# Two Fori loops of a fused attention, routing and expert kernel written out as straight code

## The chip, the core and the metric

The kernel runs on one core of one Trainium2 chip. The metric is the device time of one execution in microseconds (us). Three runs of the kernel before gave 960.48, 960.57 and 961.03 us: a median of 960.57 us.

Five engines work side by side, each through its own list of instructions: PE (matrix products; PEld is its load of weights), DVE (vector), ACT (activation), POOL (GpSimd) and SP, which only issues transfers here. They meet through semaphores: an instruction adds to one, and another waits until it has reached a value.

## The reference, cut to what matters

```python
# 1: linear attention with decay; r, k, v: (4, 8, 768, 48)
for t in range(S):
    cur = einsum('bhd,bhe->bhde', u * kt, vt)
    y[:, :, t] = einsum('bhd,bhde->bhe', rt, state + cur)
    state = w * state + einsum('bhd,bhe->bhde', kt, vt)
x = y.transpose(0, 2, 1, 3).reshape(3072, 384)

# 2: each token goes to one of 8 experts, best logit first, 384 tokens per expert
logits = x @ w_gate
for idx in argsort(-logits.flatten()):
    tok, e = idx // E, idx % E
    if assigned[tok] >= 0 or counts[e] >= cap: continue
    assigned[tok] = e; counts[e] += 1
for e in range(8):
    out[mask_e] = relu(x[mask_e] @ w1[e]) @ w2[e]      # w1: 384x1024, w2: 1024x384

# 3: a bilinear layer; w_a, w_b: 384x1536, w_out: 1536x384
return ((out @ w_a) * (out @ w_b)) @ w_out
```

## The kernel before, in words

**Attention.** The tokens are cut into 24 tiles of 128 (4 batches of 6). SP loads r, k and v of a tile three tiles ahead, and between them pieces of the third layer's weights (`raw`). Per tile PE makes scores (L981), turns the next tile (L957) and the last result (L965), makes the state's update (L991), the product with the scores (L999), the gate's logits (L971) and the product with the state (L1005). DVE scales and masks, POOL makes `ktok`, `ruk`, `sfade` and `dv` and, with ACT, splits the `raw` weights into an upper and a lower part (`w_all`). All four call the helper `all_tiles` (L300), which puts tile 0 ahead, tiles 1 to 18 in a loop of three passes of six, and tiles 19 to 23 behind it. SP does not use it: its list is written out.

**Routing.** The search for the first expert's tokens (24 products of L1026 and one of L1032, six times, with DVE between them) stands behind the attention, outside any loop. That for expert i+1 is spread between the products of expert i (`routing` on PE; `route_keys` and what follows on DVE, L636 to L766).

**Experts.** One call of `expert(i, ...)` takes one expert through its two layers and the bilinear layer. PE: L1069 (first layer, later the products with w_a and w_b), L1112 (second layer), L1143 (last product). Each result leaves in two parts: ACT writes the upper (`upper_hidden` L909, L922, L925), DVE the lower (`lower_hidden` L780, L807, L810). Meanwhile POOL gathers the next expert's weights by row number (`rows_i`, L681; L461, L465) into `wst` and takes off the upper part (L478); ACT makes the upper part of the first six pieces (L904), between its other work, in order.

**What the loops contain.** PE and DVE run experts 0 to 5 in one loop body and write out experts 6 and 7. ACT and POOL run seven passes in the loop and write out the last. In a loop body the pass number is a register, so a wait that grows from pass to pass is met by computing the value first (`REGISTER_ALU`, or `ISA` where the value is moved) and waiting for the register. The order of the work on each engine is that of the code; no scheduler moves it.

Of the kernel before, what the change touches and what calls it, by code (L numbers as in the profile page):

```python
# [16 lines left out]
def attention_moe_bilinear(nc, r, k, v, w, u, w_gate, w1, w2, w_a, w_b, w_out, out, x_rows):  # L17
    B, H, S, DH = r.shape
    D, E = w_gate.shape
# [32 lines left out]
    with ctx:  # L52
# [250 lines left out]
        def all_tiles(engine, tile):  # L303


            tile(0, 0, False)
            with engine.Fori(0, B - 1) as b:
                for j in range(1, TPB + 1):
                    tile(b, j, True)
            for j in range(1, TPB):  # L310
                tile(B - 1, j, False)
# [52 lines left out]
        def _(pool):  # L364
# [46 lines left out]
            def tile(b, j, in_loop):  # L411
# [20 lines left out]
                if in_loop and j >= 2:  # L432
                    for c, count, piece, cols in raw_pieces(j - 1):
# [7 lines left out]
                                   ALU.mult).then_inc(dv_ready, 1)  # L441

            all_tiles(pool, tile)


# [34 lines left out]
            def prepare(m, first):  # L480


                pool.wait_ge(rows_ready, m + 1)
                for k in range(CHUNKS + 2):
                    if k < CHUNKS:
                        gather_weights(m, k)
                    if k >= 2 and not (first and k - 2 in BY_DVE):
                        split_weights(m, k - 2, first)
                    if k == (TOKENS_AT_0 if first else TOKENS_AT):
                        pool.wait_ge(ids_ready, m + 1)  # L490
                        pool.wait_ge(xg_turned, 1 + m * DC)
                        pool.sem_inc(pool_go, 1)
                        for t in range(CT):
                            pool.indirect_dma_start(xg[:, t, :], None, x_rows,
                                                    bass.IndirectOffsetOnAxis(ap=ids_next[:, t:t + 1], axis=0)
                                                    ).then_inc(xg_landed[t], 16)

            def store(i):
                pool.wait_ge(now_ready, i + 1)
                for t in range(CT):  # L500
                    pool.wait_ge(os_ready, 1 + i * CT + (t + 1))
                    pool.sem_inc(pool_go, 1)
                    pool.indirect_dma_start(out, bass.IndirectOffsetOnAxis(ap=ids_now[:, t:t + 1], axis=0),  # L503
                                            os_[:, t, :], None).then_inc(o_stored, 16)
                pool.wait_ge(o_stored, i * (16 * CT) + 16 * CT)
                pool.sem_inc(o_flushed, 1)

            prepare(0, True)
            with pool.Fori(0, E - 1) as i:
                prepare(i + 1, False)  # L510
                store(i)
            store(E - 1)
# [2 lines left out]
        def _(dve):  # L515
# [53 lines left out]
            def tile(b, j, in_loop):  # L569
# [25 lines left out]
                if j >= 1:  # L595
# [3 lines left out]
                                  ALU.add).then_inc(x_ready, 1)  # L599

            all_tiles(dve, tile)


# [173 lines left out]
            def lower_hidden(i, f):  # L777

                dve.wait_ge(hs_hi, i * FC + (f + 1))
                dve.scalar_tensor_tensor(hs2[:, f % 2, 1, :], ring[f % 2][:, 0:CAP], 0.0,  # L780
                                         hs2[:, f % 2, 0, :].bitcast(F32), ALU.max, ALU.subtract
                                         ).then_inc(hs_lo, 1)
# [69 lines left out]
                dve.tensor_tensor(lo, src, hi.bitcast(F32), ALU.subtract).then_inc(w_split, 1)  # L852
            assert made[0] == CHAIN
            lower_hidden(0, 0)
            with dve.Fori(0, E - 2) as i:
                expert(i, True, True)
            expert(E - 2, True, False)
            expert(E - 1, False, False)
# [2 lines left out]
        def _(act):  # L861
# [8 lines left out]
            def tile(b, j, in_loop):  # L870
# [7 lines left out]
                if in_loop:  # L878
                    for c, count, piece, cols in raw_pieces(j):
# [5 lines left out]
                               ).then_inc(lg_ready, 1)  # L885

            all_tiles(act, tile)


# [16 lines left out]
            def upper_hidden(i, f):  # L906

                act.wait_ge(h_done, i * FC + (f + 1))
                act.activation(hs2[:, f % 2, 0, :], ring[f % 2][:, 0:CAP], ACT.Relu).then_inc(hs_hi, 1)  # L909

            def expert(i, more):
                for f in range(1, FC):
                    upper_hidden(i, f)
                for c in range(DC):
                    act.wait_ge(yt_done, i * DC + (c + 1))
                    act.activation(act2[:, 0, c, :], acc[c][:, 0:CAP], ACT.Copy).then_inc(yt_hi, 1)
                act.wait_ge(raw_lo, RAW_PIECES)
                for c in range(FFC):
                    act.wait_ge(a_part, i * FFC + (c + 1))

                    act.wait_ge(gs_lo, 1 + i * FFC + max(c - 1, 0))
                    act.activation(ga[:, c % 2, :], ring[2 * (c % 2)][:, 0:CAP], ACT.Copy).then_inc(as_ready, 1)  # L922

                    act.wait_ge(g_ready, i * FFC + (c + 1))
                    act.activation(gs2[:, c % 2, 0, :], ga[:, c % 2, :], ACT.Copy).then_inc(gs_hi, 1)  # L925
                    if more and c >= ACT_FROM:
                        for k in range(2 * (c - ACT_FROM), 2 * (c - ACT_FROM) + 2):
                            if k in BY_ACT:
                                upper_weights(i + 1, k)
                if more:  # L930
                    upper_tokens(i + 1)
                    upper_hidden(i + 1, 0)
                act.wait_ge(o_flushed, 1 + i)
                for t in range(CT):
                    act.wait_ge(o_done, i * CT + (t + 1))
                    act.activation(os_[:, t, :], acc[t][:, 0:D], ACT.Copy).then_inc(os_ready, 1)  # L936
# [5 lines left out]
                    act.wait_ge(raw_lo, RAW_PIECES)  # L942
                upper_weights(0, k)
            upper_hidden(0, 0)
            with act.Fori(0, E - 1) as i:
                expert(i, True)
            expert(E - 1, False)

# [1 line left out]
        def _(pe):  # L950
# [135 lines left out]
            def first_up(i):  # L1086

                for c in range(DC):
                    pe.wait_ge(w_split, 1 + i * CHUNKS + (c + 1) * (F // WIDE))
                    pe.wait_ge(xgt_lo, 1 + i * DC + (c + 1))  # L1090
                    for a, b in ((0, 0), (0, 1), (1, 0)):
                        last = pe.matmul(ring[0][:, 0:CAP], w1_2[:, a, c, 0:P], act2[:, b, c, :],  # L1092
                                         start=(c == 0 and (a, b) == (0, 0)),
                                         stop=(c == DC - 1 and (a, b) == (1, 0)))
                last.then_inc(h_done, 1)
# [87 lines left out]
                route_numbers(0, part)  # L1183
            turn_tokens(0)
            first_up(0)
            with pe.Fori(0, E - 2) as i:
                expert(i, True, True)
            expert(E - 2, True, False)
            expert(E - 1, False, False)
# [30 lines left out]
```

## Time and profile before

| | |
|---|---|
| median of 3 runs | 960.57 us |
| the profiled execution | 960.47 us, of which 958.7 us is the span from first to last instruction |
| PE busy | 900.8 us (94%) |
| DVE, POOL, ACT busy | 509.3, 470.3 and 218.8 us |
| chain that ended last | PE 92%, DVE 3%, POOL 2%, DMA 1%, issue 1% |
| mean granted TensorE clock | 0.967 |

Busy shares and the chain are means over stages: attention fills the first 180 us, the first routing goes on until about 231 us, and the experts take the rest.

### The profile page before, as it was taken

The page shows a single profiled execution, that of the slowest core. Times are in us where ns is not written, and L with a number is a line of the kernel's source. Part 1 is how long each engine was busy: PE and PEld are TensorE (multiplying, and loading weights), DVE is VectorE, ACT ScalarE, POOL GpSimd, SP SyncE. Part 2 cuts the span into 40 slices and gives each one's busy share as a digit, 9 for nine tenths or more (in the row PEclk, how much of TensorE's full clock was granted, in tenths as well). Part 3 has the DMA queues.
Part 4 walks back from the last instruction along what each step waited for, and adds up shares of the span by engine and source line. Part 5 has one row for each costly group of instructions (what it writes and reads, how often), then busy time and mean ns, then how long its engine had stood idle before and what let it go on. Part 6 is the DMA issues. An engine that isn't in the chain of part 4 may idle for free.

```text
span 958.7 us, 17931 instructions
## 1 busy us (share of the span) xinstructions
PE 900.8 (94%) x6581; PEld 864.6 (90%) x6581; DVE 509.3 (53%) x1238; ACT 218.8 (23%) x454; POOL 470.3 (49%) x491
## 2 busy tenths in 40 slices
PE   5999999625999999999999999999999999999995
PEld 5999999614999999999999999999999999999995
DVE  6777677576555456465636563656455532432221
ACT  0212120002113211322222223223312232222221
POOL 5988897216406731771178037604750673277001
PEclk9999999756999999999999999999999999999998
DMA  5785754003002200220121012101210121122000
GB/s 104 210 220 115 194 124 105 26 22 111 25 2 75 75 33 33 66 57 25 33 82 52 13 44 79 57 0 55 77 49 0 66 77 38 34 83 66 1 1 25
DMA packets 92782, 61.19 MB, mean 64 GB/s; under 512 B 78800, under 2 KB 83536, under 8 KB 92752
## 3 DMA queue, kind: packets, MB, share of 16 engines
q0 software_dynamic: 11008, 34.61, 11.8%
q1 hardware_dynamic: 77872, 21.45, 9.8%
q10 hardware_dynamic: 3872, 4.72, 1.4%
q8 instruction: 20, 0.33, 0.1%
q14 instruction: 10, 0.08, 0.0%
HBM read 51.33 MB, written 9.44 MB: 63 GB/s over the span
## 4 chain that ended last, share of the span: by engine, by line
PE 92%; DVE 3%; POOL 2%; issue 1%; DMA 1%; ACT 0%; SPq 0%; POOLq 0%; DVEq 0%; ACTq 0%
PE bank L1069 39%; PE bank L1143 16%; PE bank L1112 11%; PE bank L981 4%; PE bank L999 4%; PE bank L1026 3%; PE bank L957 2%; PE bank L1005 2%; PE bank L1125 2%; PE bank L991 2%; PE bank L1092 2%; PE bank L971 2%; PE bank L1129 1%; PE bank L965 1%; PE bank L1060 1%
## 5 line engine op out<-in xcount | busy, mean ns | idle before, releaser
L1069 PE MATMUL bank<-act,w_all 128*128 128x384 f32 x1584 | 298.4, 338 | 0.0
L1069 PEld LDWEIGHTS bank<-act,w_all 128*128 128x128 f32 x1584 | 274.4, 188 | 1.1
L461 POOL DMA_INDIRECT wst<-in_moe_w,rows_i x48 | 52.2, 1087 | 274.7 <-DVE rows_i L681 217.3
L1143 PE MATMUL bank<-w_all,gs 128*128 128x384 f32 x864 | 168.2, 338 | 0.3 <-DVE gs L810 0.3
L478 POOL TENSOR_TENSOR w<-wst,w 128x384 fp32r<-128x384 f32 (+1 forms) x106 | 131.0, 1236 | 43.6 <-ACT w L904 37.9
L1143 PEld LDWEIGHTS bank<-w_all,gs 128*128 128x128 f32 x864 | 149.6, 188 | 2.1 <-DVE gs L810 1.6
L807 DVE TENSOR_TENSOR ga<-ga,bank 128x384 f32<-128x384 f32 x96 | 53.1, 554 | 140.5 <-PE bank L1069 90.0
L1112 PE MATMUL bank<-hs,w 128*128 128x384 f32 x576 | 111.4, 339 | 0.6 <-DVE hs L780 0.6
L1112 PEld LDWEIGHTS bank<-hs,w 128*128 128x128 f32 x576 | 99.9, 188 | 1.4 <-issue 0.9
L1069 PE MATMUL bank<-act,w 128*128 128x384 f32 x504 | 99.0, 339 | 0.0
L465 POOL DMA_INDIRECT wst<-in_moe_w,rows_i x64 | 64.1, 1002 | 50.4 <-POOL w L478 35.8
L1069 PEld LDWEIGHTS bank<-act,w 128*128 128x128 f32 x504 | 87.8, 188 | 0.9
L925 ACT ACTIVATE gs<-ga 128x384 fp32r<-128x384 f32 x96 | 50.5, 526 | 157.3 <-DVE ga L807 157.3
L780 DVE SCALAR_TENSOR_TENSOR hs<-bank,hs 128x384 fp32r<-128x384 f32 x64 | 35.6, 557 | 92.6 <-ACT hs L909 89.0
L810 DVE TENSOR_TENSOR gs<-ga,gs 128x384 fp32r<-128x384 f32 x96 | 53.8, 560 | 56.8 <-ACT gs L925 56.8
L922 ACT ACTIVATE ga<-bank 128x384 f32<-128x384 f32 x96 | 46.7, 486 | 134.8 <-PE bank L1069 101.7
L909 ACT ACTIVATE hs<-bank 128x384 fp32r<-128x384 f32 x64 | 31.5, 492 | 170.9 <-PE bank L1069 153.5
L503 POOL DMA_INDIRECT out<-os_,ids_now x24 | 24.0, 1002 | 69.2 <-ACT os_ L936 63.2
L904 ACT ACTIVATE w<-wst 128x512 fp32r<-128x512 f32 (+1 forms) x50 | 30.4, 621 | 92.4 <-DMA wst<-in_moe_w,rows_i 92.2
L1026 PEld LDWEIGHTS bank<-mask_mem,want 128*8 128x8 bf16 x1008 | 28.9, 85 | 24.1 <-DVE mask_mem L630 15.3
L981 PE MATMUL bank<-rs,ks 128*128 128x128 f32 x384 | 49.0, 282 | 0.0
L1026 PE MATMUL bank<-mask_mem,want 128*8 128x41 bf16 x1008 | 35.4, 184 | 13.1 <-DVE mask_mem L630 13.1
(165 smaller groups left out, 1141.5 us busy)
## 6 DMA issues: line engine op xcount, KB each, us to landing
rt<-in_r SPq DMA_DIRECT2D x24, 192.0 KB, 3.0
kt<-in_k SPq DMA_DIRECT2D x24, 192.0 KB, 4.0
vt<-in_v SPq DMA_DIRECT2D x24, 192.0 KB, 4.1
x_rows<-xs ACTq DMA_DIRECT2D x24, 192.0 KB, 3.4
raw<-in_moe_w_a SPq DMA_DIRECT2D x3, 768.0 KB, 6.2
raw<-in_moe_w_b SPq DMA_DIRECT2D x3, 768.0 KB, 6.5
raw<-in_moe_w_out SPq DMA_DIRECT2D x3, 768.0 KB, 7.7
wst<-in_moe_w,rows_i POOLq DMA_INDIRECT x112
```

The lines of the kernel that those rows point to most:

```text
L461: pool.indirect_dma_start(wst[:, k % STAGES, :], None, w1_rows, bass.IndirectOffsetOnAxis(ap=rows_i[:, k:k + 1], axis=0)).then_inc(wst_lan ...
L465: pool.indirect_dma_start(wst[:, k % STAGES, 0:D], None, w2_rows, bass.IndirectOffsetOnAxis(ap=rows_i[:, k:k + 1], axis=0)).then_inc(wst_l ...
L478: pool.tensor_tensor(lo, src, hi.bitcast(F32), ALU.subtract).then_inc(w_split, 1)
L807: dve.tensor_tensor(ga[:, c % 2, :], ga[:, c % 2, :], ring[2 * (c % 2) + 1][:, 0:CAP], ALU.mult).then_inc(g_ready, 1)
L810: dve.tensor_tensor(gs2[:, c % 2, 1, :], ga[:, c % 2, :], gs2[:, c % 2, 0, :].bitcast(F32), ALU.subtract).then_inc(gs_lo, 1)
L922: act.activation(ga[:, c % 2, :], ring[2 * (c % 2)][:, 0:CAP], ACT.Copy).then_inc(as_ready, 1)
L925: act.activation(gs2[:, c % 2, 0, :], ga[:, c % 2, :], ACT.Copy).then_inc(gs_hi, 1)
L981: last = pe.matmul(pA[g][:, a, :], ks[:, a, g, :], rs[:, two, a, :], start=True, stop=True)
L1026: last = pe.matmul(pCnt, want[:, j, :], mask[:, j, :], start=(j == 0), stop=(j == NT - 1))
L1069: last = pe.matmul(dst, wt(a), mv(b), start=(n == 0 and (a, b) == (0, 0)), stop=(n == len(pairs) - 1 and (a, b) == (1, 0)))
L1112: last = pe.matmul(acc[c][:, 0:CAP], w2_2[:, a, f, c * P:c * P + P], hs2[:, f % 2, b, :], start=(f == 0 and (a, b) == (0, 0)), stop=(f == ...
L1143: last = pe.matmul(acc[t][:, 0:D], gs2[:, c % 2, a, t * P:t * P + P], wo2[:, b, c, :], start=(c == 0 and (a, b) == (0, 0)), stop=(c == FFC ...
```

## The change

The four uses of `Fori` become Python's `for`, so that the bodies are laid out once per pass and every number in them is a constant.

```diff
 def all_tiles(engine, tile):
             tile(0, 0, False)
-            with engine.Fori(0, B - 1) as b:
+            for b in range(B - 1):
                 for j in range(1, TPB + 1):
                     tile(b, j, True)
             for j in range(1, TPB):
@@ pool
-            with pool.Fori(0, E - 1) as i:
+            for i in range(E - 1):
                 prepare(i + 1, False)
                 store(i)
@@ dve
-            with dve.Fori(0, E - 2) as i:
+            for i in range(E - 2):
                 expert(i, True, True)
@@ act
-            with act.Fori(0, E - 1) as i:
+            for i in range(E - 1):
                 expert(i, True)
@@ pe
-            with pe.Fori(0, E - 2) as i:
+            for i in range(E - 2):
                 expert(i, True, True)
```

In the built programs PE has 2423 instructions before and 6162 now (a matrix product counted once), DVE 677 and 1421, POOL 310 and 764, ACT 259 and 617, SP 125 in both.

The first place is PE at the end of the attention loop's body, tile 6 on to tile 7. Before:

```order
L989 REGISTER_ALU
L991 MATMUL bank<-vt,ktok 128x96 [waits ktok_ready]
L991 MATMUL bank<-vt,ktok 128x96 x3
L996 REGISTER_ALU
L999 MATMUL bank<-vt,am 128x48 [waits x_ready,am_ready]
L999 MATMUL bank<-vt,am 128x48 x7
L971 MATMUL bank<-gate_w,xt 128x8 [waits xt_ready]
L971 MATMUL bank<-gate_w,xt 128x8 x2
L307 REGISTER_ALU
L307 COMPARE_AND_BRANCH
```

Now, at the same place:

```order
L991 MATMUL bank<-vt,ktok 128x96 [waits ktok_ready]
L991 MATMUL bank<-vt,ktok 128x96 x3
L999 MATMUL bank<-vt,am 128x48 [waits x_ready,am_ready]
L999 MATMUL bank<-vt,am 128x48 x7
L971 MATMUL bank<-gate_w,xt 128x8 [waits xt_ready]
L971 MATMUL bank<-gate_w,xt 128x8 x2
L981 MATMUL bank<-rs,ks 128x128 [waits am_ready,scaled]
```

The register work and the branch are gone, and the next tile's scores (L981) follow at once. The matrix products and their order are the same.

The second place is DVE at the start of an expert: `route_keys` (L639 to L651) for the next expert, then the lower part of the hidden values (L780). Before:

```order
L639 TENSOR_TENSOR lm<-logit,lid 128x192
L622 ISA
L640 TENSOR_REDUCE key<-lm 128x24 [waits dve_step]
L622 REGISTER_ALU
L643 TENSOR_SCALAR code<-key 128x24 [waits dve_step]
L644 TENSOR_TENSOR lm<-lm,key 128x192
L622 REGISTER_ALU
L645 TENSOR_TENSOR code<-code,key 128x24 [waits dve_step]
L646 TENSOR_TENSOR want<-lm,is_open 128x192
```

Now, at the same place:

```order
L639 TENSOR_TENSOR lm<-logit,lid 128x192
L640 TENSOR_REDUCE key<-lm 128x24 [waits dve_step]
L643 TENSOR_SCALAR code<-key 128x24 [waits dve_step]
L644 TENSOR_TENSOR lm<-lm,key 128x192
L645 TENSOR_TENSOR code<-code,key 128x24 [waits dve_step]
L646 TENSOR_TENSOR want<-lm,is_open 128x192
```

Nothing has changed places; the same operations wait for the same semaphores, without register work between them.

## Rows read from the trace of the kernel before

**Rows 1.** The page's chain that ended last, share of the span by engine.

```profile
PE 92%; DVE 3%; POOL 2%; issue 1%; DMA 1%; ACT 0%; SPq 0%; POOLq 0%; DVEq 0%; ACTq 0%
```

**Rows 2.** Waits of PE from 239 us on, summed over the rest.

```profile
PE bank L1112 <- DVE hs L780: 0.6, 1, 0.6
PE bank L1143 <- DVE gs L810: 0.3, 1, 0.3
```

**Rows 3.** Windows of one expert's length: length, busy time per engine, PEclk, DMA share, GB/s.

```profile
258.83:350.20 91.37, 91.37 (x656) 86.71 (x655) 50.86 (x132) 23.21 (x48) 42.82 (x42) 1.00 0.16 48
350.20:441.59 91.39, 91.39 (x656) 86.71 (x655) 50.85 (x132) 23.21 (x48) 42.82 (x42) 1.00 0.16 47
441.59:533.15 91.56, 91.56 (x656) 86.73 (x655) 50.02 (x132) 23.21 (x48) 42.51 (x42) 1.00 0.16 47
804.15:887.83 83.68, 83.68 (x504) 82.58 (x504) 30.31 (x71) 23.23 (x47) 41.56 (x42) 1.00 0.17 53
```

**Rows 4.** DMA queues of the whole run: packets, MB, share of 16 engines.

```profile
q8 instruction: 20, 0.33, 0.1%
q14 instruction: 10, 0.08, 0.0%
```

**Rows 5.** DMA queues, window 258.83 to 350.20.

```profile
q8 instruction: 4, 0.07, 0.3%
```

**Rows 6.** DMA queues, window 350.20 to 716.27; no other queue is listed.

```profile
q0 software_dynamic: 5504, 17.31, 15.5%
```

**Rows 7.** DMA queues, window 20 to 62 in the attention.

```profile
q1 hardware_dynamic: 19440, 7.47, 69.1%
q8 instruction: 3, 0.05, 0.5%
```

**Rows 8.** Timeline: start, length, engine, line, operation, [idle before]. Short routing products, in the loop and written out.

```profile
289.49 0.10 PEld L1042 LDWEIGHTS bank<-tot,before 128*128 128x128 bf16 x1 [0.16 <-issue]
332.50 0.65 PEld L1026 LDWEIGHTS bank<-mask_mem,want 128*8 128x8 bf16 x24 [0.25 <-issue]
830.51 0.10 PEld L1042 LDWEIGHTS bank<-tot,before 128*128 128x128 bf16 x1 [0.16 <-issue]
```

**Rows 9.** Timeline of the attention: starts of tiles 7, 8, 13 and 14.

```profile
61.02 2.03 PE L981 MATMUL bank<-rs,ks 128*128 128x128 f32 x16
68.31 1.98 PE L981 MATMUL bank<-rs,ks 128*128 128x128 f32 x16
102.62 2.03 PE L981 MATMUL bank<-rs,ks 128*128 128x128 f32 x16
104.96 0.42 PEld L957 LDWEIGHTS bank<-ident,rt 128*128 128x128 f32 x4 [0.51 <-DMA vt<-in_v]
110.44 1.75 PE L981 MATMUL bank<-rs,ks 128*128 128x128 f32 x14
```

**Rows 10.** Timeline of expert 0: DVE's `route_keys` beside POOL's split, and PE behind them.

```profile
236.26 0.70 DVE L645 TENSOR_TENSOR code<-code,key 128x24 int32<-128x24 int32 x1
237.00 1.11 POOL L478 TENSOR_TENSOR w<-wst,w 128x384 fp32r<-128x384 f32 x1
237.26 0.88 DVE L647 TENSOR_SCALAR code<-code 128x24 int32<-128x24 int32 x1
239.34 1.53 PEld L1112 LDWEIGHTS bank<-hs,w 128*128 128x128 f32 x9 [0.87 <-issue]
```

**Rows 11.** The same DVE operation in the first routing, where POOL is idle.

```profile
185.79 0.18 DVE L645 TENSOR_TENSOR code<-code,key 128x24 int32<-128x24 int32 x1
```

**Rows 12.** Timeline of expert 2: a gather that lands, ACT, then DVE and PE behind it.

```profile
491.00 0.63 ACT L904 ACTIVATE w<-wst 128x512 fp32r<-128x512 f32 x1 [3.25 <-DMA wst<-in_moe_w,rows_i]
493.80 1.52 PEld L1143 LDWEIGHTS bank<-w_all,gs 128*128 128x128 f32 x9 [0.26 <-DVE gs L810]
```

**Rows 13.** Window just before the clock's rise; columns as in rows 3.

```profile
232.00:234.00 2.00, 2.00 (x8) 2.00 (x7) 1.17 (x3) 0.53 (x2) 0.94 (x1) 0.50 0.05 18
```

**Rows 14.** A piece of the chain at the low clock: start, length, engine, line, count.

```profile
230.76 3.23 PE bank L1092 x9
```

## The prediction

> **What bounds the kernel now.** I read the chain that ended last first: 92% of the span is PE [rows 1]. The second view is the list of PE's waits. After 239 us the whole expert stage holds two waits, 0.6 and 0.3 us [rows 2]. So a change that only makes sequencers lighter can win no more than the few places where PE is late, plus the time in which PE is busy by the record but paced by its own instruction stream. The third view looks for the latter: windows of one expert's length. In each window of the loop PE is busy for its whole length, 91.37, 91.39 and 91.56 us, and in the written-out expert 6 for 83.68 us of 83.68 [rows 3]. Last I read the DMA queues, for the instruction packets, because more code is the one thing that the change adds.
>
> **The change part by part.**
>
> *Branches.* Of PE's branches that are taken back, two go in the attention (after tiles 6 and 12) and five in the expert loop. What they cost now is read off passes that contain one. The windows of rows 3 each hold one back edge of PE (near 326, 417 and 508 us), and PE is idle in none of them. Tile 7, the first after a back edge, starts at 61.02 and the next at 68.31, 7.29 us apart with no idle time put down to PE [rows 9]. Value 0. Bound: what rows 2 and 9 leave, under 0.1 us each.
>
> The trace shows instruction packets only where code is met for the first time: the window 258.83 to 350.20 has 4 packets on q8 [rows 5], and the next four passes list no instruction queue at all [rows 6]. The Trainium skill (Runtime: NRT & Kernel Launch, Instruction fetch mechanics) says that a taken branch whose target lies outside the fetched window stalls until its page is brought in, and counts this as a reason to unroll. By that rule the loop should have a packet and a stall in each pass; the trace doesn't agree, since the passes are repeated without any packet. What it would give if it did hold is the first rival.
>
> *Register work and waits on registers.* On PE it stands ahead of the short routing products. Those are preceded by a pause of 0.25 us of the weight load for L1026, in the loop [rows 8]. Is it the register? L1042 is the control, since it is in the loop at 289.49 and written out at 830.51: the pause is 0.16 us in both [rows 8]. I take 0 for the register, and give the pause to the change from long to short products. The 0.09 us between 0.25 and 0.16 has no control, as L1026 and L1032 exist written out only in the first routing, where they wait for DVE. Bounds: 0 to -0.09 us x 12 x 6 experts = -6.5 us; 0 is the nearer, because the control shows none.
>
> On DVE the register work stands between the steps of `route_keys`. In expert 0 this is where PE is late: L780 waits behind them, and PE's weight load for L1112 has stood idle for 0.87 us [rows 10]. But what stretches the steps there is not registers: L645 took 0.70 us and L647 0.88 beside POOL's split at 237.00 [rows 10], and L645 takes 0.18 us where POOL is idle [rows 11]. Written-out code keeps POOL's split at the same place. Value 0; bounds 0 and -0.9, the whole wait. On ACT and POOL register work hides under PE, which is what they wait for.
>
> *The two places where PE waits for something else.* (a) Tile 13 takes 110.44 - 102.62 = 7.82 us where tile 7 took 7.29: 0.5 us is lost to the late landing of a `vt` load, with `raw` loads queued before it [rows 9]. That load is issued when tile 11's `dv` is done, behind POOL's and ACT's splits of `raw`, which lose a register step each. I let them come some tenths earlier and the 0.5 us go: -0.5. Bounds -0.5 and, if an instruction packet now stands in front of the load, +1.1 (the price of a packet is worked out below). (b) From expert 2 on a pass is 91.56 and not 91.38: in it PE waits 0.26 us for DVE's `gs`, which waits for ACT, which stood in its queue behind a weight piece whose gather landed at about 491.0 [rows 12, 3]. Some 0.18 us in each of four passes, 0.7 in all. The start of the gathers depends on DVE's chain, which gets slightly shorter. I take a third of it, -0.2; bounds -0.7 and 0.
>
> *More code to fetch.* PE has 2423 instructions in the program before and 6162 after. Its queue should be q8, with 20 packets [rows 4]; by the ratio some 51 of 16 KB after, and q14 some 22 in place of 10. That is 31 x 16 KB + 12 x 8 KB = 0.6 MB beside 61 MB: as bandwidth nothing. As a stall: in the window 258.83 to 350.20 the body is met for the first time, with 4 packets on q8, and PE loses 0.02 us less than in the pass without packets; expert 6, also new code, has PE busy without a gap; and tiles 1 to 6 run at full pace with 3 packets on q8 while the loads keep the DMA engines at 69.1% [rows 3, 5, 7]. So fetching ahead covers it. As contention: 4 packets take 0.3% of 16 engines in 91.37 us, 4.4 us, so 1.1 us each [rows 5]. A gather that meets one on its DMA engine lands up to that much later, and the one of rows 12 has no slack left. ACT stands idle 3.25 us for it [rows 12]; 4 packets in 91 us fall into such a stretch in about one pass of seven, and by half of their length on average: 5 passes x 1/7 x 0.55 = +0.4. Not each shares the gather's engine, so I take +0.3.
>
> *Sum:* branches 0, registers 0, tile 13 -0.5, gathers -0.2, packets +0.3 = -0.4 us. The profiled execution took 960.47 us (span 958.7, some 1.8 around it, which doesn't change); the sum gives **960.1 us**. The median of the runs shown is 960.57, 0.1 above that execution, within their spread.
>
> **The rivals.**
>
> *Branches are dear after all.* Two back edges in the attention and five in the expert loop, each with one packet of 1.1 us to wait for: -7.7, 952.8 us. For it: nothing in the rows; PE is idle at none of the seven. 2%.
>
> *Waits on registers pace PE.* The 0.09 us of the short products goes, -6.5, and with it 953.6 us. For it: the pause is longer just at the products that exist only in the loop. Against it: L1042 in the loop. 5%.
>
> *Packets delay the gathers.* Place: ACT's L904, which waits for the gather and holds `ga` and `gs` behind it, in passes 1 to 5, which have no packets now [rows 6, 12]. Price: 1.1 us per pass if the packet of each pass always stands before that gather, 5 x 1.1 = 5.5, less the 0.7 gained elsewhere: 965.3 us. The passes are equally long, but a packet comes every 250 or so instructions and a pass isn't a whole number of them, so the place shifts; it decides from three meetings in five, 3 x 1.1 - 0.7 = +2.6. Against it: expert 0 met four packets at no cost, and expert 6 is level too. 8%.
>
> *The change doesn't do what it says:* if it left waits on registers, the time would be that of before; it would not be told from my forecast.
>
> **How the numbers follow.** My forecast has 83%, the rivals 2, 5 and 8, and 2 are left for what I don't see. 0.2%, or 1.9 us, is about what a measurement of this kernel can tell from no change; that is 958.6 to 962.5. Within the forecast the terms' bounds are -0.5 to +1.1 for tile 13, -0.9 to 0 for expert 0, -0.7 to 0 for the gathers. To these comes PE's clock: the granted clock was 0.50 until about 234 us, and nine products took 3.23 us there [rows 13, 14], while nine take 9 x 83.68 / 504 = 1.5 us at the full level [rows 3]; if it rises one such group sooner or later, the time moves by 1.7 either way. Together these make 958.4 to 961.9, the range, outside which the rivals lie. Faster by over 0.2%: 0.02 + 0.05 + 0.03 from the forecast's lower end = 0.10. Slower: 0.08. Within: 0.82.
>
> **What would show it.** Right: 50 or so packets on q8; passes of 91.3 to 91.6 us with PE busy throughout; the pause before L1042 0.16 and before L1026 still 0.25 us; tile 13 near 7.3. Wrong: a pause of 0.16 before L1026 (the second rival); PE waits for DVE's `gs` of 1 us in several passes (the third); PE idle where a packet lands.

## The result, and the profile after

The changed kernel is slower, by little: 962.56 us median against 960.48 for the kernel before on the same chip (15 runs each), ratio 1.0023 with a 95% interval of 1.0015 to 1.0031, which is 1.4 to 3.0 us. I had forecast 960.1. The profiled execution took 962.83 us against 960.47, so it shows 2.36 us to explain.

I read the same views in the same order. First the queues of the whole run and the chain that ended last, from the page:

```profile
q8 instruction: 52, 0.85, 0.4%
q14 instruction: 23, 0.19, 0.1%
...
PE 88%; DVE 4%; POOL 2%; issue 2%; DMA 2%; ACT 1%; POOLq 0%; DVEq 0%; ACTq 0%
```

The packets came as worked out (52 and 23 for the forecast 51 and 22; before 20 and 10 [rows 4]). The chain has left PE for 4% more of the span than before [rows 1]. Where it did so, the windows of one expert's length tell. Each begins at the same place of a pass, some 22.5 us behind an expert's first L1112, and is named after the expert in which it begins; columns as in rows 3:

```profile
258.67:350.24 91.57, 91.57 (x655) 86.74 (x655) 50.21 (x132) 23.20 (x48) 42.82 (x42) 1.00 0.17 48
350.24:441.83 91.59, 91.56 (x655) 86.71 (x655) 50.84 (x132) 23.20 (x48) 42.74 (x42) 1.00 0.16 48
...
716.35:806.09 89.74, 88.11 (x580) 84.86 (x581) 40.54 (x103) 23.11 (x47) 42.01 (x42) 1.00 0.16 49
806.09:890.25 84.16, 83.68 (x505) 82.54 (x504) 30.62 (x71) 23.21 (x47) 42.17 (x42) 1.00 0.18 52
```

The same window of expert 5 before, for the third of these (for the fourth it is in rows 3, 83.68):

```profile
716.27:804.15 87.88, 87.88 (x581) 84.88 (x581) 39.49 (x103) 23.12 (x47) 41.78 (x42) 1.00 0.16 49
```

Expert 5 starts 0.08 us later than before (716.35 against 716.27) and ends 1.94 later. Expert 6 adds 0.48. So hardly anything is spread over the loop: one pass is 1.86 us longer, with PE idle in it for 1.63, and the next is 0.48 longer. The list of PE's waits for 239 to 961 us names what it waited for:

```profile
PE bank L1143 <- DVE gs L810: 1.7, 3, 0.9
PE bank L1092 <- DVE act L774: 0.7, 1, 0.7
```

Before, the first of these was 0.3 us and the second wasn't there; the 0.6 us of L1112 in rows 2 is gone now. The next rows are the timeline of expert 5 after the change, from the gather of ACT's sixth and last piece of weights to the product that is late (start, length, engine, line, operation, idle before and what ended it):

```profile
761.59 1.74 POOL L461 DMA_INDIRECT wst<-in_moe_w,rows_i  x1 [0.81 <-POOL w L478]
...
766.73 0.63 ACT L904 ACTIVATE w<-wst 128x512 fp32r<-128x512 f32 x1 [4.21 <-DMA wst<-in_moe_w,rows_i]
767.27 0.47 ACT L922 ACTIVATE ga<-bank 128x384 f32<-128x384 f32 x1
767.77 0.56 DVE L807 TENSOR_TENSOR ga<-ga,bank 128x384 f32<-128x384 f32 x1 [3.10 <-ACT ga L922]
...
768.91 0.56 DVE L810 TENSOR_TENSOR gs<-ga,gs 128x384 fp32r<-128x384 f32 x1 [0.59 <-ACT gs L925]
...
769.52 1.52 PEld L1143 LDWEIGHTS bank<-w_all,gs 128*128 128x128 f32 x9 [1.24 <-DVE gs L810]
```

The same ACT instruction before, on ACT's timeline:

```profile
765.61 0.63 ACT L904 ACTIVATE w<-wst 128x512 fp32r<-128x512 f32 x1 [3.18 <-DMA wst<-in_moe_w,rows_i]
```

The gather was issued at 761.59, and at 761.52 before. ACT began 5.14 us behind it (766.73), before 4.09, so the piece is 1.05 us late; `ga`, `gs` and PE stand behind it. In that stretch the DMA view of the changed kernel has an instruction packet of PE's queue. The first row is of the window 761.0 to 767.2, the second of 763.5 to 764.0, which has nothing else in it:

```profile
q8 instruction: 1, 0.02, 1.2%
```

```profile
q8 instruction: 1, 0.02, 15.1%
```

15.1% of 16 engines for 0.5 us is 1.2 us of one engine. By the single packets of the trace it starts at 763.92, 0.15 us ahead of the gather's first data; these took 2.18 us from first to last, where the other six passes of this kernel took 1.2 to 1.65.

The second loss follows at the end of the same pass. First the changed kernel, then the one before:

```profile
780.39 1.01 POOL L478 TENSOR_TENSOR w<-wst,w 128x384 fp32r<-128x384 f32 x1
780.41 1.40 DVE L810 TENSOR_TENSOR gs<-ga,gs 128x384 fp32r<-128x384 f32 x1 [0.59 <-ACT gs L925]
...
782.40 1.53 PEld L1092 LDWEIGHTS bank<-act,w 128*128 128x128 f32 x9 [1.00 <-POOL w L478]
```

```profile
779.33 0.56 DVE L810 TENSOR_TENSOR gs<-ga,gs 128x384 fp32r<-128x384 f32 x1 [0.59 <-ACT gs L925]
779.42 0.82 POOL L476 CAST w<-wst 128x384 fp32r<-128x384 f32 x1
...
780.32 1.01 POOL L478 TENSOR_TENSOR w<-wst,w 128x384 fp32r<-128x384 f32 x1
780.47 1.52 PEld L1092 LDWEIGHTS bank<-act,w 128*128 128x128 f32 x9 [0.16 <-issue]
```

PE, ACT and DVE come 1 us late to the end of the pass, POOL doesn't. Its subtraction now starts 0.02 us ahead of DVE's instead of 0.99 behind it, and DVE's takes 1.40 us in place of 0.56. PE's weight load stands for 1.00 us in place of 0.16. With the piece's 1.05 that is 1.05 + 0.84 = 1.89, the pass's 1.86. The wait list gives the same by the matmuls, 0.9 and 0.7 us, the window's 1.63 of idle PE.

### The profile page after: what moved, and what is told of

It reads as the page before. It is cut to its first block, busy times and chain, and to the rows that moved or that the text cites. A ratio compares the mean times of both kernels' runs of the same rounds, so it can differ in the third digit from the quotient of the medians.

```text
span 961.1 us, 16277 instructions
## 1 busy us (share of the span) xinstructions
PE 902.4 (94%) x6581; PEld 866.0 (90%) x6581; DVE 512.0 (53%) x1238; ACT 218.8 (23%) x454; POOL 471.8 (49%) x491
## 4 chain that ended last, share of the span: by engine, by line
PE 88%; DVE 4%; POOL 2%; issue 2%; DMA 2%; ACT 1%; POOLq 0%; DVEq 0%; ACTq 0%
PE bank L1069 36%; PE bank L1143 14%; PE bank L1112 11%; PE bank L981 5%; PE bank L999 4%; PE bank L1026 3%; PE bank L957 2%; PE bank L1005 2%; PE bank L1125 2%; PE bank L991 2%; PE bank L971 2%; PE bank L1092 2%; POOL w L478 1%; DMA wst<-in_moe_w,rows_i 1%; PE bank L1129 1%
## 5 line engine op out<-in xcount | busy, mean ns | idle before, releaser
L1069 PE MATMUL bank<-act,w_all 128*128 128x384 f32 x1584 | 298.5, 339 | 0.0
L1069 PEld LDWEIGHTS bank<-act,w_all 128*128 128x128 f32 x1584 | 274.4, 188 | 1.2
L1143 PE MATMUL bank<-w_all,gs 128*128 128x384 f32 x864 | 168.2, 338 | 1.7 <-DVE gs L810 1.7
L1143 PEld LDWEIGHTS bank<-w_all,gs 128*128 128x128 f32 x864 | 149.7, 188 | 3.9 <-DVE gs L810 3.8
L1112 PE MATMUL bank<-hs,w 128*128 128x384 f32 x576 | 111.3, 339 | 0.0
L1112 PEld LDWEIGHTS bank<-hs,w 128*128 128x128 f32 x576 | 100.0, 188 | 0.6
L1069 PE MATMUL bank<-act,w 128*128 128x384 f32 x504 | 99.9, 342 | 0.0
L1069 PEld LDWEIGHTS bank<-act,w 128*128 128x128 f32 x504 | 88.7, 190 | 0.9
L810 DVE TENSOR_TENSOR gs<-ga,gs 128x384 fp32r<-128x384 f32 x96 | 55.4, 577 | 56.8 <-ACT gs L925 56.8
L780 DVE SCALAR_TENSOR_TENSOR hs<-bank,hs 128x384 fp32r<-128x384 f32 x64 | 35.6, 557 | 91.8 <-ACT hs L909 91.3
L1026 PEld LDWEIGHTS bank<-mask_mem,want 128*8 128x8 bf16 x1008 | 28.9, 85 | 24.1 <-DVE mask_mem L630 16.0
L981 PE MATMUL bank<-rs,ks 128*128 128x128 f32 x384 | 49.3, 284 | 0.0
L1026 PE MATMUL bank<-mask_mem,want 128*8 128x41 bf16 x1008 | 35.4, 184 | 13.1 <-DVE mask_mem L630 13.1
```

Source lines behind the costliest of these rows:

```text
L810: dve.tensor_tensor(gs2[:, c % 2, 1, :], ga[:, c % 2, :], gs2[:, c % 2, 0, :].bitcast(F32), ALU.subtract).then_inc(gs_lo, 1)
L981: last = pe.matmul(pA[g][:, a, :], ks[:, a, g, :], rs[:, two, a, :], start=True, stop=True)
L1026: last = pe.matmul(pCnt, want[:, j, :], mask[:, j, :], start=(j == 0), stop=(j == NT - 1))
L1069: last = pe.matmul(dst, wt(a), mv(b), start=(n == 0 and (a, b) == (0, 0)), stop=(n == len(pairs) - 1 and (a, b) == (1, 0)))
L1112: last = pe.matmul(acc[c][:, 0:CAP], w2_2[:, a, f, c * P:c * P + P], hs2[:, f % 2, b, :], start=(f == 0 and (a, b) == (0, 0)), stop=(f == ...
L1143: last = pe.matmul(acc[t][:, 0:D], gs2[:, c % 2, a, t * P:t * P + P], wo2[:, b, c, :], start=(c == 0 and (a, b) == (0, 0)), stop=(c == FFC ...
```

## The experiments

Theory A: the loss is one PE packet in front of that gather, in one pass, and the collision at the pass's end behind it. Rival B: the written-out code itself slows an engine. Lines in kernels with an edit can be up to three off: L1142 and L1145 are L1143, L1091 and L1094 are L1092, L1068 is L1069, L813 is L810. A ratio compares with the kernel before on the same chip, whose median was 960.16 us for the first four experiments, 959.26 for the next four and 959.97 for the last four; none of the differences is over 0.3% but that of the kernel with 480 waits, so read the intervals.

**PE's expert loop back to a loop, all else written out.**

```
-            for i in range(E - 2):
+            with pe.Fori(0, E - 2) as i:
                 expert(i, True, True)
```

> The changed kernel, with PE's expert loop alone put back as a loop; DVE, ACT, POOL and the attention stay written out. Theory A (PE's instruction packets delay a weight gather that ACT, DVE and PE then wait for): hardly any q8 packets in the passes of the search experts, no wait of PE for gs over 0.35 us there, ratio to before 1.000 (960.5 us). Theory B (the written-out DVE, ACT and POOL code shifts the gathers or their users so that PE waits): the loss stays, ratio 1.002 (962.5 us). Theory C (spread of the gathers alone, no packets in it): also unchanged from the written-out kernel, 1.002.

Measured: 960.14 against 960.16 us, ratio 0.9997 (0.9987 to 1.0007). Its page and its expert 5:

```profile
q8 instruction: 26, 0.43, 0.2%
...
715.15:803.19 88.04, 88.04 (x580) 84.87 (x581) 39.66 (x103) 23.14 (x47) 41.60 (x42) 1.00 0.17 49
```

With the 26 packets gone the long pass is gone, PE busy for all of it. The loops of ACT, DVE and POOL and the whole attention stay written out and cost nothing.

**PE's expert loop alone written out.**

```
-            with pe.Fori(0, E - 2) as i:
+            for i in range(E - 2):
                 expert(i, True, True)
```

> The kernel before, with PE's expert loop alone written out; all other loops stay. Theory A: some 47 packets on q8, PE late at L1143 by about 1 us in one or two passes, ratio 1.001 to 1.002 (961.5 to 962.5 us). Theory B: as before, 1.000 (960.5 us).

Measured: 962.61 us, ratio 1.0015 (1.0006 to 1.0025). Waits of PE's weight load between 625 and 890 us:

```profile
PEld bank L1143 <- DVE gs L810: 2.1, 2, 1.0
PEld bank L1092 <- POOL w L478: 2.0, 2, 1.0
```

PE's code alone is enough. Here experts 5 and 6 are both hit (89.51 and 85.21 us): packets start 0.42 us ahead of the gather's data in the one and 0.01 behind its start in the other.

**The attention alone written out.**

```
-            with engine.Fori(0, B - 1) as b:
+            for b in range(B - 1):
```

> The kernel before, with the attention loop alone written out on all four engines; the expert loops stay. Theories A and B both put the loss into the experts: ratio 0.999 to 1.000 (960.0 to 960.5 us), tile 13 shorter by 0.3 us, no pause at other tiles. A rival D puts it into the attention (packets beside the loads, a later rise of the clock): 1.001 to 1.002.

Measured: 960.43 us, ratio 1.0004 (0.9994 to 1.0013): nothing. Its expert 6 took 84.33 us, 0.65 more than before, without an instruction packet within 6 us of that gather. In the waits of PE's weight load between 625 and 890 us the first row is what stands at this pass's end:

```profile
PEld bank L1092 <- POOL w L478: 1.0, 1, 1.0
PEld bank L1143 <- DVE gs L810: 0.7, 2, 0.4
```

DVE's subtraction took 1.36 us there, behind POOL's. So the collision of POOL and DVE at the end of a pass also comes without a packet.

**All written out, and ACT's sixth piece later.** If theory A holds, the cure is slack and not fewer packets. The piece is split after product group 8 in place of 7.

```
-                    if more and c >= ACT_FROM:
-                        for k in range(2 * (c - ACT_FROM), 2 * (c - ACT_FROM) + 2):
-                            if k in BY_ACT:
-                                upper_weights(i + 1, k)
+                    if more:
+                        for k in {5: (0, 1), 6: (2, 3), 7: (4,), 8: (5,)}.get(c, ()):
+                            upper_weights(i + 1, k)
```

> The changed kernel, but ACT makes the upper part of weight piece 5 one product later (after the upper parts of product 8 instead of those of product 7), so that a late gather of it holds nothing back. Theory A: q8 still has 52 packets, PE's waits for gs at L1143 vanish (0.3 us in most passes, 1 us in one), ratio 0.999 to 1.000 (959.5 to 960.5 us). Theory D (loss elsewhere than at this gather): 1.0015 to 1.002 (962 to 962.5 us). A knock-on on POOL (piece 5 is split 3 us later) would show as a wait of PE at L1092 for POOL or DVE, up to 1 us per pass: 1.005.

Measured: 958.35 us, ratio 0.9978 (0.9969 to 0.9987). Expert 5, and ACT in it, `ga` and then the sixth piece:

```profile
714.25:801.95 87.70, 87.70 (x581) 84.90 (x581) 39.35 (x103) 23.14 (x47) 41.83 (x42) 1.00 0.16 50
```

```profile
760.29 0.47 ACT L922 ACTIVATE ga<-bank 128x384 f32<-128x384 f32 x1
...
764.77 0.63 ACT L904 ACTIVATE w<-wst 128x512 fp32r<-128x512 f32 x1 [1.25 <-DMA wst<-in_moe_w,rows_i]
```

The packet still comes, 0.36 us after the gather's first data, and the data take 2.41 us, the longest of all these kernels. But that `ga` is 4.48 us ahead of the piece and PE loses nothing: same 52 packets, same meeting, no loss. By the ratio it is 2.1 us faster than the kernel before, more than theory A explains (below).

**The changed kernel again.**

> The changed kernel itself once more, as the neighbour of the next three on one chip. Theory A (a PE instruction packet in front of the gather of weight piece 5): ratio 1.002 again, and the pass with the packet 47 to 49 us after its start (expert 5) 1 to 2 us longer than the others. Theory C (gathers spread on their own): 1.002 too, but the long pass is another one.

Measured: 961.08 against 959.26 us, ratio 1.0018 (1.0009 to 1.0027). Expert 5 is the long one again:

```profile
715.92:805.33 89.41, 88.12 (x581) 84.86 (x581) 40.39 (x103) 23.16 (x47) 41.68 (x42) 1.00 0.16 49
```

Its packet starts 0.20 us ahead of the gather's data, in the first run 0.15. Two profiled executions of one program thus met in the same place, 0.05 us apart. Expert 6 took 83.43 us this time, in the first profile 84.16. The executions without a profile can't tell: the changed kernel's first fifteen spread from 960.09 to 963.69 us, the kernel before's from 958.84 to 961.23, so it isn't excluded that some of them escape the meeting.

**The code moved by idle instructions.** 240 waits on PE that are already fulfilled, before the first tile, and 240 before the first tokens; then another kernel with 56, only before the tokens.

```
+            for _ in range(240):
+                pe.wait_ge(s_cpool, CP_CAUSAL)
             turn_tokens(0)
```

> The changed kernel with 240 more PE instructions that do nothing (waits already met) where PE is idle: half before the attention, half while PE waits for the first tokens. A packet brings 256 instructions, so all packets come later by 16 instructions, some 1.4 us against the work: the one of expert 5 at 48.8 us in place of 47.4, behind the gather's last data, and none of experts 1 to 5 lies at 46.4 to 48.6. Theory A: no wait of 1 us for gs in experts 1 to 5, ratio 1.000 to 1.001 (960.3 to 961.3 us). Theories B and C: as the changed kernel, 1.002 or more (the extra instructions can only add).

> The changed kernel with 28 more PE instructions that do nothing, while PE waits for the first tokens. All packets of the experts come some 2 us earlier against the work: that of expert 4 moves from 49.7 to 47.7 us after its start, into the gather of piece 5, that of expert 5 to 45.4, before it. Theory A: the long pass is expert 4 and no longer 5, ratio 1.001 to 1.003. Theories B and C: expert 5 stays the long one (B), or no rule (C).

Measured: 976.52 us, ratio 1.0178 (1.0165 to 1.0192), with 480; 961.67 us, ratio 1.0022 (1.0012 to 1.0033), with 56. Of the first kernel two of PE's waits before 300 us, and its expert 5; of the second, experts 5 and 6:

```profile
PE bank L957 <- issue: 17.5, 1, 17.5
PE bank L1062 <- issue: 13.3, 1, 13.3
```

```profile
732.66:820.38 87.72, 87.72 (x580) 84.89 (x581) 39.43 (x103) 23.16 (x47) 41.87 (x42) 1.00 0.16 50
```

```profile
715.12:804.23 89.11, 88.11 (x580) 84.86 (x581) 40.43 (x103) 23.15 (x47) 41.41 (x42) 1.00 0.16 50
804.23:889.38 85.15, 83.82 (x504) 82.54 (x504) 31.19 (x71) 23.25 (x47) 41.89 (x42) 1.00 0.17 52
```

The expectations count instructions (240 and 28) where the kernels got twice as many waits (480 and 56); whether two such waits make one instruction isn't shown, the first kernel has one packet more on q8 (53). I missed the total of the first, and the ratio of the second fell into what I expected, but not its long passes. The first wait was 6.6 us and the second 5.9 in the changed kernel; the idle instructions themselves cost that kernel its 17 us, so its ratio says nothing. From the window of expert 0 to the end of that of expert 6, though, it took 628.43 us, the changed kernel 631.58 and the one before 629.00: no pass is hit; the packets come 1.21 us (expert 5) and 0.77 us (expert 6) behind the gather's first data. With 56 the packet of expert 5 moved by only 0.4 us, to 0.58 ahead, so expert 5 stayed long, and the next one moved into expert 6's gather (0.43 ahead). The place decides, then; how far a given number of instructions moves it I could not forecast.

The meetings of all these kernels beside each other, from the single packets of the trace. "Packet" is its start from the gather's first data, "data" the time from first to last, "PE idle" the time without a matrix product in the 50 us from the pass's first gather on:

```
kernel, expert                    packet   data   PE idle
changed, 5                        -0.15    2.18   1.63
changed, 6                        +1.65    1.65   0.48
changed again, 5                  -0.20    2.01   1.29
changed again, 6                  +1.07    1.19   0.00
PE alone written out, 5           -0.42    2.03   1.38
PE alone written out, 6           +0.01    2.06   1.41
56 waits more, 5                  -0.58    1.78   1.00
56 waits more, 6                  -0.43    2.01   1.33
480 waits more, 5                 +1.21    1.25   0.00
480 waits more, 6                 +0.77    1.12   0.00
changed, 4                        +2.24    1.26   0.00
PE in a loop, 5                   none     1.36   0.00
late piece, 5                     +0.36    2.41   0.00
late piece, 6                     +1.45    1.45   0.00
late piece again, 5               +0.06    2.11   0.00
late piece, PE alone out, 5       +0.14    2.20   0.00
late piece, PE alone out, 6       -0.46    2.10   0.00
```

A packet that starts between 0.6 us ahead of the first data and 0.4 behind goes with data times of 1.8 to 2.4 us, ten times out of ten. In all other passes of all 14 traces they are 1.1 to 1.65, mostly under 1.4, and passes without any packet near reach 1.6 too. In nine of the ten meetings, and in no other pass, three or four of the gather's 80 packets stand by themselves, over 0.25 us behind the others. That fits one of the 16 DMA engines being held by the instruction packet; the trace doesn't name a packet's engine, so this last step is inferred. With the piece late, PE doesn't notice: four hits, no idle time.

**Before, with the late piece alone.** Is the gain of the best version that of the late piece?

> The kernel before, loops and all, with ACT's piece 5 one product later, as in e4. Theory A: the small waits for gs (0.2 to 0.3 us in most passes) go: ratio 0.998 to 0.999 (958.4 to 959.5 us), and the two kernels with the later piece are equal within 0.1%, so that with slack at this gather written-out code costs nothing. If written-out code had a cost or a gain of its own, the two would differ by it: Theory E (constants win 1 us that the packets hid): 0.999 to 1.000 here, over 0.1% above e4.

Measured: 959.91 us, ratio 1.0007 (0.9998 to 1.0016). No gain, and my expectation failed. Its five passes from the window of expert 0 on took 91.5 to 91.6 us where the written-out kernel's took 91.3 (one 91.37). Locating the 0.3 us took the timeline at the end of a pass, here of expert 3:

```profile
595.11 0.51 POOL L476 CAST w<-wst 128x384 fp32r<-128x384 f32 x1
595.23 0.81 DVE L810 TENSOR_TENSOR gs<-ga,gs 128x384 fp32r<-128x384 f32 x1 [0.59 <-ACT gs L925]
...
595.97 1.47 DVE L774 TENSOR_TENSOR act<-bank,act 128x384 fp32r<-128x384 f32 x3
596.62 1.54 PEld L1091 LDWEIGHTS bank<-act,w 128*128 128x128 f32 x9 [0.41 <-issue]
```

POOL's copy starts 0.12 us ahead of DVE's subtraction, which then takes 0.81 us in place of 0.56, and PE waits 0.41 in place of 0.16. It is so at all seven ends of passes, with 0.77 to 0.91 us for the subtraction. In the written-out kernel with the late piece the copy comes 0.1 us behind it at six of seven, and the subtraction takes 0.56. It is the collision of expert 5 above on a smaller scale, and the trace gives its rule: in all 21 places of the 14 traces where POOL's copy or subtraction was running when this subtraction started, and ran on for more than 0.2 us, DVE ended 0.41 to 0.43 us after POOL did (here POOL at 595.62, DVE at 596.04; in expert 5 above POOL at 781.40, DVE at 781.81). DVE doesn't share, it waits for the end of POOL's operation. Two theories remained for the 0.3 us: this order (O), or the back edges (L). Four kernels on one chip tell them apart.

**The same, with the order forced.**

```
                 pool.sem_inc(pool_go, 1)
+                if k == 7 and not first:
+                    pool.wait_ge(gs_lo, 1 + m * FFC)
+                    pool.sem_inc(pool_go, 1)
                 src, hi, lo = parts_of(k)
```

> The looped kernel with ScalarE's late sixth piece, and one wait more: GpSimd begins its copy of the eighth piece of weights (CAST, L476) only when VectorE has ended its last subtraction of the pass (L810). In the run without this wait the copy came 0.1 us ahead of that subtraction at every end of a pass, the subtraction took 0.77 to 0.91 us in place of 0.56, the gap before TensorE's first L1091 of the pass was 0.55 to 0.70 in place of 0.35, and passes took 91.57 to 91.59. Theory O (the order of these two at the pass's end makes the 0.3 us per pass, not the loops' back edges): passes of 91.3, gap 0.35, ratio 0.998 against before. Rival L (the loops' own branches and register operations make it): passes stay 91.55 to 91.6 although the gap goes to 0.35 or not, ratio 1.000 to 1.001.

Measured: 958.47 against 959.97 us, ratio 0.9983 (0.9975 to 0.9992). A pass of the loop, and its end:

```profile
441.18:532.49 91.31, 91.31 (x655) 86.77 (x655) 51.77 (x132) 23.20 (x48) 43.08 (x42) 1.00 0.15 47
```

```profile
595.35 0.56 DVE L813 TENSOR_TENSOR gs<-ga,gs 128x384 fp32r<-128x384 f32 x1 [0.59 <-ACT gs L928]
...
596.08 0.51 POOL L479 CAST w<-wst 128x384 fp32r<-128x384 f32 x1 [0.61 <-DVE gs L813]
...
596.50 1.53 PEld L1094 LDWEIGHTS bank<-act,w 128*128 128x128 f32 x9 [0.16 <-issue]
```

All passes of the loop are 91.29 to 91.31 us, with all loops in place. Theory O holds: on top of the late piece, one wait on POOL is worth 0.3 us a pass, and back edges nothing. The wait without the late piece was not run.

**Late piece, with PE's loop alone written out; late piece, with PE's loop alone kept; the best version again.**

> The looped kernel with ScalarE's late sixth piece and TensorE's expert loop alone written out (q8 near 46 packets). If the 0.3 us per pass of the kernel with everything written out is TensorE's own back edge: passes of 91.3, ratio 0.998. If it is the order of GpSimd's copy and VectorE's subtraction at the end of a pass: whichever order this version falls into decides, 91.3 with VectorE first, 91.55 to 91.6 with GpSimd first. In both theories no pass of 89 us for the expert after the last search, since the late piece is hidden.

> Everything written out and the sixth piece late, but TensorE's expert loop a loop again (q8 near 26 packets). If TensorE's back edge costs the 0.3 us per pass: passes of 91.57, ratio 1.000. If the loops of the other engines did: passes of 91.3, ratio 0.998. If it is the order of copy and subtraction: the passes with VectorE first 91.3, the others 91.55 to 91.6, with either ratio.

> The same kernel as the one with everything written out and the late sixth piece, again, on this chip: ratio 0.998 (0.997 to 0.999) against before, VectorE first at every end of a pass, passes of 91.3, q8 52 packets. If it was chance or the chip, 0.999 to 1.001 and passes of 91.55 to 91.6.

Measured: 958.18 us, ratio 0.9982 (0.9973 to 0.9991); 958.40 us, 0.9981 (0.9973 to 0.9990); 958.70 us, 0.9984 (0.9976 to 0.9993). A pass of the kernel with PE's loop written out, then of the one that keeps it:

```profile
440.55:531.85 91.30, 91.30 (x656) 86.75 (x655) 50.75 (x132) 23.23 (x48) 42.74 (x42) 1.00 0.16 48
```

```profile
439.45:530.75 91.30, 91.30 (x655) 86.76 (x655) 51.77 (x132) 23.20 (x48) 42.74 (x42) 1.00 0.16 48
```

So with slack for the sixth piece and the good order, it is the same whether PE's loop is written out or not, and whether the others' are. In all three DVE is first at every end. At one end (411 us of the kernel with PE's loop) the subtraction took 0.73 us all the same, and the pass, from L1091 to L1091, 91.48. So the order of the starts isn't all of it, but the subtraction's length and the pass's go together here too. Why the loop kernel with the late piece fell into the other order, and these three did not, is open; each was profiled once, the best version twice.

## Why the prediction was wrong

*Branches and registers, 0.* Right. The pause before L1026 is 0.25 us in the changed kernel too, and before L1042 0.16:

```profile
277.09 0.65 PEld L1026 LDWEIGHTS bank<-mask_mem,want 128*8 128x8 bf16 x24 [0.25 <-issue]
...
289.32 0.10 PEld L1042 LDWEIGHTS bank<-tot,before 128*128 128x128 bf16 x1 [0.16 <-issue]
```

Both rivals that rested on sequencers fall, and the loop with forced order shows it from the other side: 91.3 us a pass with the back edge. (Their times were not counted from one base: 952.8 and 965.3 start from the 960.5 of the kernel before, 953.6 from the forecast.)

The Trainium skill's rule that a taken branch beyond the fetched window stalls (Runtime: NRT & Kernel Launch, Instruction fetch mechanics) is not seen at PE's back edge: with it and without it a pass takes 91.30 us, by the windows of the kernels with the late piece. But the prediction drew too much from it. The same section of the Trainium skill gives PE's instruction memory room for 2048 instructions, in blocks of 256, beside the window of two pages. A pass of PE is about five such blocks, by the 26 packets that five passes more bring, so by the size of the memory the body fits and no packet is due in a repeated pass. The trace agrees with that size, and not with a window of two pages.

*Tile 13, -0.5.* Half of it: the wait for `vt` is 0.21 us in place of 0.51, and the tile takes 7.53 in place of 7.82. Nothing of it is left at the routing: tile 13 itself starts 0.68 us later than before (103.30 and 102.62), since tile 0 took 7.6 us in place of 6.7, and near 200 us the two kernels are within 0.02 us of each other.

```profile
105.35 0.42 PEld L957 LDWEIGHTS bank<-ident,rt 128*128 128x128 f32 x4 [0.21 <-DMA vt<-in_v]
```

*Expert 0 and the clock.* The wait of 0.87 us [rows 10] is gone, yet expert 0's window starts only 0.16 us earlier (258.67 and 258.83). The two go together. The granted clock rose later. The first pair of rows is of the kernel before, the second of the changed one, each a window and then the first layer's products (L1069) that the rise falls into:

```profile
234.00:235.50 1.50, 1.50 (x9) 1.50 (x9) 0.93 (x3) 0.49 (x1) 0.99 (x2) 0.96 0.47 127
233.78 1.89 PE L1069 MATMUL bank<-act,w 128*128 128x384 f32 x9
```

```profile
234.00:235.50 1.50, 1.50 (x6) 1.50 (x5) 1.12 (x3) 0.31 (x1) 1.18 (x2) 0.50 0.47 131
233.58 2.74 PE L1069 MATMUL bank<-act,w 128*128 128x384 f32 x9
```

At 0.50 the nine products took 0.85 us longer, so PE came late enough to find `hs` ready. It isn't the written-out code that removed the wait: the kernel with PE in a loop and all else written out, whose clock was at 1.00 by 233.5 us, still has 0.8 us of it. I had the clock as an uncertainty of 1.7 us either way; its later rise cost what the wait gave back.

*Gathers, -0.2.* Wrong in sign, small: the first five passes of the loop sum to 716.35 - 258.67 = 457.68 us, before to 716.27 - 258.83 = 457.44. I had given the 0.2 us more of passes such as the third [rows 3] to a late gather [rows 12]. In the kernel before, these three are also the ones that end with POOL's copy ahead of DVE's subtraction, so the order is a rival to that reading. The trace decides for the gather: at that end the subtraction took 0.58 or 0.59 us in place of 0.56 and PE's weight load stood for 0.18 or 0.19 in place of 0.16, while at L1143 there is up to 0.26 us [rows 12]. The copy was 0.35 us ahead there and nearly done. In the kernel with PE in a loop the passes without any wait at L1143 took 91.3 us, loops or not.

*Packets, +0.3: the step that failed.* Its parts were right: 52 packets, five in a pass where four were counted, one of them 1.2 us long (1.1 priced), in front of a gather without slack, which delays ACT, then `ga` and `gs`, then PE by 1.0 us. The size was wrong in two ways. First the chance. "Once in seven passes, by half of its length" averages over places as if each execution drew anew. But expert 5 was met in both profiles of the changed kernel and in four of the five other programs with PE's loop written out, from 0.58 us ahead to 0.36 behind; only the 480 idle instructions moved it away. In a given program the profiled meetings stand at the same place, I take it because fetching and gathers both follow PE's progress (argued, not shown by itself). The cost is then near 0 or near the full 1.1, and my mean was neither. Second, what is behind it. I priced PE's wait as the end of the matter, but an engine that comes late meets others in new places: POOL's subtraction, on time, now ran beside DVE's, and this added 0.8 us. So the term, put at 0.3, measured 1.0 + 0.8 in expert 5, and with the 0.5 of expert 6 that is the 2.3 us of the two profiles' difference.

*The third rival* (packets delay the gathers, 965.3 us) had the mechanism, the engine and the line. But it decided from three meetings in five passes; one meeting, made double by the collision, was enough to cross the line. Against it stood expert 0, which met four packets at no cost. That showed only that these four were elsewhere: the nearest starts 5.8 us ahead of that gather's data.

*The range* ended at 961.9. It held the bounds of the other terms and one mean of this one, not its full hit with what follows. Nor did it hold the bounds in full. With all of them at one end they make 957.0 to 963.6, which would have held the result by luck of its width; how they were put together to 958.4 to 961.9 isn't stated.

Left open: expert 6's 0.48 us in the changed kernel. Its gather's data took 1.65 us with a packet starting only at their end (+1.65), so that packet doesn't explain it. In the second profile of the same program the data took 1.19 us and PE lost nothing.

## What to carry to other kernels

Price a contention that may repeat with the program as hit and as not hit, not by its mean alone, and add what the late engine runs into next. Where the list of waits shows a transfer with no slack, give it slack before adding anything that uses the same DMA engines: moving one piece by one product group took away the whole loss, with all 52 packets still there. And before writing loops out, check what the back edges cost. Here they cost nothing, and the 1.5 us that were to be had (ratio 0.9983) took two steps with all loops in place: the slack for that piece, which alone brought nothing, and one wait that sets the order in which two engines start at the end of a pass.

## What I had not expected of the hardware

- DVE's 128x384 subtraction takes 0.56 us alone, 0.77 to 0.91 when POOL's copy starts just ahead of it, and 1.36 to 1.40 when POOL's whole subtraction does. It ends 0.41 to 0.43 us after POOL's operation, in 21 of 21 places. Started first, DVE keeps its 0.56 (0.63 and 0.73 at two ends) and POOL's copy takes up to 0.82 in place of 0.51.
- One 16 KB instruction packet (0.9 to 1.4 us) that starts within 0.6 us ahead and 0.4 us behind a gather's first data goes with data of 1.8 to 2.4 us, in ten of ten meetings, in place of about 1.3.
- 240 waits on PE that were already fulfilled left a gap of 17.5 us ahead of the first L957, where the changed kernel has 6.6.
